# Top-32 attention with two gated feed-forward stages: five places for split output chunks, weight slices one per slot, an early copy on ScalarE, and the experts' first parts between the tail's copies

## Chip, cores and metric

The kernel runs on one core of a Trainium2 chip. The metric is the time of one execution in device microseconds (us), the median of several runs. All data is float32.

## The reference

```python
# attention: q, k, v of [2, 8, 576, 64]
scores = scale * np.matmul(q, k.transpose(0, 1, 3, 2))
kth = np.partition(scores, -32, axis=-1)[..., -32:-31]
scores = np.where(scores >= kth, scores, -1000000000.0)
attn = softmax(scores);  x = attn @ v          # laid out as [1152, 512]
# gated stage: w_a, w_b of [512, 1536], w_out of [1536, 512]
x = ((x @ w_a) * (x @ w_b)) @ w_out
# four experts: w1 of [512, 1024], w2 of [1024, 512] each
p = domain_probs / (domain_probs.sum(-1, keepdims=True) + 1e-09)
out = sum over e of p[:, e:e + 1] * (np.maximum(x @ w1[e], 0.0) @ w2[e])
```

## The kernel before

**Split operands.** The large products run on rounded operands: a tensor is split into an upper part (a ScalarE copy with rounding) and a lower part (whole minus upper, on GpSimd or VectorE), and a product is three matmuls: upper by upper, upper by lower, lower by upper.

**Attention and gated stage, slots 0 to 40.** The 1152 tokens are 9 tiles of 128 (`NT`), the 8 heads 4 pairs (`PR`), which makes 36 pairs of a tile and two heads (`NP`). A loop of slots `n` = 0 to 40 (`LAST`) runs on all engines. In slot n VectorE searches the 32 largest scores of pair n (`top_scores`: per head four MAX8 and three MATCH_REPLACE8, 14 operations, with small work placed between them by `between`). GpSimd makes the limits of pair n-1 (`limits`) and subtracts (`push_down`), ScalarE makes `below_top` and the exponentials, PE transposes (`p_transpose`) and multiplies by v (`weighted_sum`). When the four pairs of a tile are done, VectorE sums and inverts (`sums`), PE turns and spreads the inverses, and VectorE scales the tile (`scale`, operation 10 of the slot, for tile 0 operation 1). The gated stage lags by 5 slots (`LAG_AB`): in slot n PE does the two products `up` of unit n-5, `h_transpose` of unit n-6 behind GpSimd's `product`, and `send` of unit n-7 (nine matmuls of 512 columns with three chunks of w_out). Units 31 to 35 run in the slots 36 to 40 and behind them, without attention beside them: the tail.

**Weights.** w_a and w_b come in eight slices (`SLICES`) by way of three places `w_raw`. Slice i is split by ScalarE (`slice_hi`, L826) in the slot that `HIGH_IN` gives and by GpSimd (L1289 to L1294) in the slot of `LOW_IN`. The twelve chunks of w_out come to `wo_raw` (`RAWS` places), are split in the slots of `CHUNKS_IN` (`chunk_hi`, L831, and L1297 to L1300) into `wo` (`RING` places), written to `wo_d` in DRAM (`keep_chunk`), and read back for each later tile (`reload_chunk`).

**Experts.** 32 steps (`STEPS`): four experts, two groups of tokens, four parts. A step is seven products (`seven`) and `downs`. Step 0 needs the first parts: `w1` parts 0 and 1 split in two instructions each (`w1_high_raws`, `w1_high_sums`, then `w1_low_part` on VectorE), the tokens `x2` in four pieces, and `w2` part 0 (`w2_high`, `w2_low`). PE's order in step 0 is `h_transpose(35)`, `p1 p5 p6 p2 p3 p7`, `send(35)`, `p4`; `p2` waits for ScalarE's eviction of `p1`, `p7` for VectorE's `u2`.

**What sets the order.** Each engine has one instruction stream, written out by hand, and waits on semaphores in that order. SP issues nearly all DMAs, also in order, so a wait of SP holds back all loads behind it.

## Time and profile before

| | |
|---|---|
| median of 3 runs | 818.04 us (817.95 to 818.12) |
| profiled execution, its own time | 818.3 us |
| its span, first to last instruction | 816.5 us |
| PE busy | 775.7 us (95%) |
| VectorE busy | 572.5 us (70%) |
| ScalarE busy | 420.6 us (52%) |
| GpSimd busy | 354.5 us (43%) |
| mean granted TensorE clock | 0.969 |

The page of the profile names the engines PE (TensorE), DVE (VectorE), ACT (ScalarE), POOL (GpSimd) and SP. Busy time is a mean over stretches with different bounds, so the views by stretch and in order of time matter more here. The number in brackets behind a row of a timeline is the idle time of the engine before it, and the arrow names what ended it. The granted clock (PEclk) is the share of full speed: 1.00 is 2.4 GHz, 0.50 is 1.2 GHz.

### The profile page before, as it was taken

How to read it: one execution, taken by the hardware profiler on the slowest of the kernel's cores; microseconds unless marked ns; L12 is line 12 of the kernel's file. 1: busy time of each engine (PE TensorE's matmuls, PEld its weight loads, DVE VectorE, ACT ScalarE, POOL GpSimd, SP SyncE). 2: the span in 40 equal slices, each digit the busy share in tenths (PEclk: the TensorE clock that was granted, in tenths of full speed). 3: DMA queues.
4: the chain of work that ended last, by engine and by line, in shares of the span. 5: the costliest groups of instructions: out<-in, count | busy, mean ns of one | idle time of the engine just before them, and what ended most of it. 6: DMA issues, size and time to landing. Idle time of an engine off the chain costs nothing.

```text
span 816.5 us, 13995 instructions
## 1 busy us (share of the span) xinstructions
PE 775.7 (95%) x5081; PEld 681.4 (83%) x5081; DVE 572.5 (70%) x1145; ACT 420.6 (52%) x818; POOL 354.5 (43%) x322
## 2 busy tenths in 40 slices
PE   4658899999999999999998999999999999999998
PEld 3437778888888888888897898999899999989997
DVE  6989999999999999997627853562455444364423
ACT  3767767777777777776554522342134322343210
POOL 3878775555444444445424302462135521464100
PEclk7569999999999999999999999999999999999999
DMA  7430668444544664544677001300032002210101
GB/s 267 144 118 17 217 230 278 160 166 163 169 169 168 213 226 169 168 156 168 209 247 228 1 26 53 104 27 1 26 104 78 1 1 78 65 65 1 52 1 65
DMA packets 53764, 97.92 MB, mean 120 GB/s; under 512 B 5696, under 2 KB 28992, under 8 KB 53696
## 3 DMA queue, kind: packets, MB, share of 16 engines
q1 hardware_dynamic: 53408, 96.76, 35.3%
q8 instruction: 41, 0.67, 0.3%
q10 hardware_dynamic: 288, 0.26, 0.1%
q14 instruction: 27, 0.22, 0.1%
HBM read 86.00 MB, written 11.01 MB: 119 GB/s over the span
## 4 chain that ended last, share of the span: by engine, by line
PE 83%; DVE 8%; POOL 4%; ACT 3%; issue 2%; ACTq 0%; POOLq 0%; DVEq 0%
PE ps L718 24%; PE ps L650 21%; PE ps L579 15%; PE ps L564 8%; PE ps L528 4%; PE ps L492 4%; PE ps L505 3%; DVE m L1020 2%; PE ps L537 2%; DVE work L1026 2%; POOL wa_lo L1293 1%; POOL p_sb L1250 1%; DVE work L1014 1%; POOL wb_lo L1293 1%; DVE m L1008 1%
## 5 line engine op out<-in xcount | busy, mean ns | idle before, releaser
L1020 DVE MAX8 m<-work 128x8 f32<-128x576 f32 x216 | 152.3, 747 | 0.0
L650 PE MATMUL ps<-x_hi,w_hi 128*128 128x256 f32 (+1 forms) x448 | 133.0, 297 | 3.2 <-DVE u_sb L1128 2.4
L718 PE MATMUL ps<-w_lo,h_hi 128*128 128x512 f32 x288 | 112.8, 392 | 0.0
L718 PE MATMUL ps<-w_hi,h_lo 128*128 128x512 f32 x288 | 112.7, 391 | 0.0
L718 PE MATMUL ps<-w_hi,h_hi 128*128 128x512 f32 x288 | 112.6, 391 | 0.0
L1250 POOL TENSOR_TENSOR p_sb<-s_sb,p_sb 128x576 f32<-128x576 f32 x72 | 101.5, 1428 | 11.7 <-ACT p_sb L770 11.7
L1026 DVE MATCH_REPLACE8 work<-m,work 128x576 f32<-128x576 f32 x144 | 106.0, 743 | 0.0
L1315 POOL TENSOR_TENSOR u_sb<-u_sb,p_sb 128x256 f32<-128x256 f32 (+1 forms) x32 | 31.6, 986 | 161.8 <-DVE u_sb L1141 161.8
L1148 DVE TENSOR_TENSOR c_sb<-ps,p_sb 128x256 f32<-128x256 f32 (+1 forms) x32 | 14.7, 458 | 120.9 <-PE ps L650 120.9
L650 PEld LDWEIGHTS ps<-x_hi,w_hi 128*128 128x128 f32 x448 | 84.6, 189 | 5.4 <-DVE u_sb L1128 2.8
L882 ACT ACTIVATE h_hi<-c_sb 128x256 fp32r<-128x256 f32 (+1 forms) x32 | 14.2, 444 | 120.7 <-DVE c_sb L1148 120.7
L650 PE MATMUL ps<-x_hi,w_raw_lo 128*128 128x256 f32 (+1 forms) x256 | 75.7, 296 | 0.0
L650 PE MATMUL ps<-x_raw_lo,w_hi 128*128 128x256 f32 (+1 forms) x256 | 75.6, 295 | 0.0
L1262 POOL TENSOR_TENSOR hT_lo<-hT_raw,hT_hi 128x384 fp32r<-128x384 f32 x36 | 36.4, 1012 | 86.6 <-ACT hT_raw L813 86.6
L1269 POOL TENSOR_TENSOR h_sb<-a_sb,b_sb 128x384 f32<-128x384 f32 x36 | 37.1, 1031 | 80.3 <-issue 79.8
L564 PE MATMUL ps<-wo,hT_hi 128*128 128x512 f32 x216 | 71.1, 410 | 0.0
L882 ACT ACTIVATE h_hi<-u_sb 128x256 fp32r<-128x256 f32 (+1 forms) x64 | 28.5, 445 | 81.0 <-POOL u_sb L1315 51.0
L1274 POOL TENSOR_TENSOR w_lo<-w_raw,w_hi 128x1024 fp32r<-128x1024 f32 x16 | 39.8, 2488 | 56.1 <-ACT w_hi L863 56.1
L764 ACT ACTIVATE s_sb<-ps 128x576 f32<-128x576 f32 x72 | 46.0, 641 | 34.9 <-POOL p_sb L1250 32.4
L718 PEld LDWEIGHTS ps<-w_hi,h_lo 128*128 128x128 f32 x288 | 54.1, 188 | 11.8
L718 PEld LDWEIGHTS ps<-w_lo,h_hi 128*128 128x128 f32 x288 | 54.1, 188 | 10.7
L718 PEld LDWEIGHTS ps<-w_hi,h_hi 128*128 128x128 f32 x288 | 54.1, 188 | 10.7
(115 smaller groups left out, 2005.8 us busy)
## 6 DMA issues: line engine op xcount, KB each, us to landing
wo<-wo_d SPq DMA_DIRECT2D x96, 512.0 KB, 5.0
w_raw<-moe_w_in SPq DMA_DIRECT2D x32, 256.0 KB, 3.2
w_raw<-moe_w_in SPq DMA_DIRECT2D x16, 512.0 KB, 4.9
wo_d<-wo SPq DMA_DIRECT2D x12, 512.0 KB, 4.5
w_raw<-moe_w_a_in SPq DMA_DIRECT2D x4, 768.0 KB, 5.1
w_raw<-moe_w_b_in SPq DMA_DIRECT2D x4, 768.0 KB, 4.4
wo_raw<-moe_w_out_in SPq DMA_DIRECT2D x12, 256.0 KB, 5.0
x_d<-x_out_sb SPq DMA_DIRECT2D x9, 256.0 KB, 2.4
```

Source lines behind the costliest of these rows:

```text
L564: mm = nc.tensor.matmul(ps_y[:, :], h[:, i, :], wo[g % RING][:, w, :], start=first and j == 0, stop=last and j == 2)
L579: mm = nc.tensor.matmul(bank[:, 0:FS], x[:, t % 2, c, :], w[:, c, cols], start=c == 0 and i == 0, stop=c == DK - 1 and i == 2)
L650: mm = nc.tensor.matmul(ps[:, bank, 0:NH[g]], w, x, start=first and c == n == 0, stop=last and c == HK - 1 and n == 2, skip_group_check=True)
L718: mm = nc.tensor.matmul(ps[:, DOWN_BANKS[j], 0:DM], h[:, f, tok], w[:, f, :], start=m == f == n == 0, stop=m == FM - 1 and f == 1 and n == 2)
L764: copy(s_sb[:, (2 * n + head) % 4, :].rearrange("p (a c) -> p a c", a=2), ps_sc[head], ACT.Copy).then_inc(ac_s, 1)
L882: copy(h_parts[k % 2][0][:, f, j * n:(j + 1) * n], src, ACT.Relu).then_inc(done, 1)
L1020: nc.vector.max(m8[:, par, i, 8 * r:8 * r + 8], work[:, i, :]).then_inc(ve_top, 1)
L1026: nc.vector.match_replace(work[:, i, :], m8[:, par, i, 8 * r:8 * r + 8], work[:, i, :], LOWEST).then_inc(ve_top, 1)
L1250: nc.gpsimd.tensor_tensor(p_sb[:, head, :], s_sb[:, (2 * n + head) % 4, :], p_sb[:, head, :], ALU.subtract).then_inc(po_p, 1)
L1262: nc.gpsimd.tensor_tensor(hT_lo[:], hT_raw[:], hT_hi[:].bitcast(F32), ALU.subtract).then_inc(po_hl, 1)
L1269: nc.gpsimd.tensor_tensor(h_sb[:], a_sb[:], b_sb[:], ALU.mult).then_inc(po_h, 1)
L1274: nc.gpsimd.tensor_tensor(lo[:], whole[:], hi[:].bitcast(F32), ALU.subtract).then_inc(po_w2, 1)
```

## The change

- `RING` 4 to 5 and `RAWS` 5 to 8: five places for split chunks, eight for their sources, four of which lie in the memory of batch 1's v. The wait of chunk 4's load for a slice goes, and v of batch 1 is loaded in slot 10, right behind k, instead of slot 11.
- Slice 0 is copied on ScalarE before the loop; the slots 0 to 3 copy (1, 2), (3, 4), 5, 6, all behind `p_out`; GpSimd's low parts are (0, 1), (2, 3), 4, 5, 6, 7 in the slots 0 to 5.
- The first two of a slot's three chunks are split at the head of the slot on ScalarE, and ahead of `hidden_low` on GpSimd; the third on ScalarE behind `p_out`.
- A tile `zero` is cleared first; PE's eight warming matmuls use it, nine more run ahead of the first `up`, and ScalarE copies it once into `invT` before anything else.
- `sums(1)` moves from operation 1 of slot 9 to operation 12 of slot 8.
- In the tail ScalarE's copies of the experts' first parts are spread: `w1` sums of part 0 behind `b_sb`, `w2_high(0)` in slot 38, pieces of `x2` one at a time, both halves of `w1` part 1 in slot 40 instead of behind the loop. GpSimd makes `w2_low(0)` in two halves in slots 39 and 40, so that `po_w2` counts one more.

```diff
@@ -81,7 +81,6 @@
         p_row = p_sb[:].rearrange("p h s -> p (h s)")
-        top[0] += 4 * H * D
         att_end = top[0]
@@ -95,6 +94,7 @@
         pick = sb("pick", [P, P])
+        zero = sb("zero", [P, P])
@@ -112,15 +112,14 @@
-        RAW, RING, RAWS = 3, 4, 5
+        RAW, RING, RAWS = 3, 5, 8
         ring_at = top[0]
...
         kt1_at = att_at + 4 * PR * S
-        wo_raw = [at(f"wo_raw{i}", [P, DM], F32, (kt1_at if i < 4 else ring_at + 8 * DM * RING - 16 * DM) + 4 * DM * i)
-                  for i in range(RAWS)]
-        assert 16 * DM <= 4 * PR * S
-        top[0] = ring_at + max(4 * DK * FS * RAW, 8 * DM * RING + 4 * DM)
+        wo_raw = [at(f"wo_raw{i}", [P, DM], F32, kt1_at + 4 * DM * i if i < 4 else v1_at + 4 * DM * (i - 4)) for i in range(RAWS)]
+        assert 16 * DM <= 4 * PR * S and 4 * DM * (RAWS - 4) <= 4 * (KC - 1) * H * D
+        top[0] = ring_at + max(4 * DK * FS * RAW, 8 * DM * RING)
@@ -157,8 +156,7 @@
         hi_at += 2 * W2B
-        u2_sb = at("u2_sb", [P, NH[1]], F32, hi_at)
-        assert hi_at + TEMP <= att_end
+        assert hi_at <= att_end
@@ -177,7 +175,9 @@
         late_at += 2 * W2B
+        u2_sb = at("u2_sb", [P, NH[1]], F32, inv_at + TEMP)
         u3_sb = at("u3_sb", [P, NH[1]], F32, inv_at)
+        assert 2 * TEMP <= 4 * DM + 16 * TOP_K
         c21_sb = at("c21_sb", [P, NH[1]], F32, late_at)
@@ -278,7 +278,7 @@
         LAG_AB = 5
-        WARM = 8
+        WARM, FILL = 8, 9
         LAST = NP + LAG_AB - 1
@@ -305,8 +305,8 @@
         SLICES = [(w, c) for c in range(PR) for w in range(2)]
-        HIGH_IN = {0: (0, 1), 1: (2, 3), 2: (4, 5), 3: (6,), 4: (7,)}
-        LOW_IN = {0: (0,), 1: (1, 2), 2: (3, 4), 3: (5,), 4: (6,), 5: (7,)}
+        HIGH_IN = {0: (1, 2), 1: (3, 4), 2: (5,), 3: (6,)}
+        LOW_IN = {0: (0, 1), 1: (2, 3), 2: (4,), 3: (5,), 4: (6,), 5: (7,)}
         CHUNKS_IN = {6: (0, 1, 2), 7: (3, 4, 5), 8: (6, 7, 8), 9: (9, 10, 11)}
@@ -362,9 +362,7 @@
             def load_chunk(g):
-                if g == 4:
-                    sp.wait_ge(po_w, 6)
-                elif g >= RAWS:
+                if g >= RAWS:
                     sp.wait_ge(po_wo, g - RAWS + 1)
@@ -374,7 +372,8 @@
                 sp.wait_ge(pe_w, g - RING + 1)
-                sp.wait_ge(st_wo[g % RING], 16 * (min(g - RING, FO - 1) // RING + 1))
+                for c in {g % FO, min(g - RING, FO - 1)}:
+                    sp.wait_ge(st_wo[c % RING], 16 * (c // RING + 1))
                 sp.dma_start(wo[g % RING][:].rearrange("p a n -> p (a n)").bitcast(F32), wo_d[g % FO]).then_inc(ld_wo[g % RING], 16)
@@ -414,7 +413,6 @@
                     sp.dma_start(kT[:, 1, :, :], k[1].rearrange("r p s -> p r s")).then_inc(ld_k1, 16)
-                if n == 11:
                     load_v(1)
@@ -512,7 +510,7 @@
                     pe.wait_ge(ld_v[0], 48)
-                    pe.wait_ge(ve_z, 3)
+                    pe.wait_ge(ve_z, 4)
                 if n == SPLIT * PR:
@@ -580,10 +578,12 @@
+            def zeros(bank, count):
+                for i in range(count):
+                    nc.tensor.matmul(bank[:, 0:P], zero[:], zero[:], start=True, stop=True)
+
             pe.wait_ge(ve_z, 1)
-            for i in range(WARM):
-                nc.tensor.matmul(ps_b[:, 0:P], x_inv[:].rearrange("p r h -> p (r h)"), x_inv[:].rearrange("p r h -> p (r h)"),
-                                 start=True, stop=True)
+            zeros(ps_b, WARM)
             scores(0)
@@ -619,6 +619,7 @@
                 if m == 0:
+                    zeros(ps_y, FILL)
                     pe.wait_ge(po_xT, 1)
@@ -694,7 +695,7 @@
                 if f == 0 and j == 0 and g == 0:
-                    pe.wait_ge(po_w2, FM * e + m + 1)
+                    pe.wait_ge(po_w2, FM * e + m + 2)
                 if m == 0 and f == 0:
@@ -910,12 +911,17 @@
             load_first_q()
+            act.wait_ge(ve_z, 1)
+            copy(invT[:], zero[:], ACT.Copy)
             scores_out(0, 0)
             scores_out(0, 1)
+            slice_hi(0)
             for n in range(LAST + 1):
...
                     x_hi(0)
+                for g in CHUNKS_IN.get(n, ())[0:2]:
+                    chunk_hi(g)
                 if j is not None:
@@ -934,46 +940,47 @@
                     h_out(u)
+                if m is not None:
+                    act.wait_ge(pe_a, m + 1)
+                    act.wait_ge(po_h, m)
+                    copy(a_sb[:], ps_a[:, 0:FS], ACT.Copy).then_inc(ac_a, 1)
                 if n == NP + 1:
...
                     w1_high_raws(0)
-                    w1_high_sums(0)
                 if n == NP + 2:
-                    x2_high_piece(0, 0)
+                    w2_high(0)
+                if n == NP + 3:
                     x2_high_piece(0, 1)
-                if n == NP + 3:
-                    x2_high_piece(0, 2)
-                    x2_high_piece(0, 3)
-                    w2_high(0)
-                for g in CHUNKS_IN.get(n, ()):
-                    chunk_hi(g)
-                if m is not None:
-                    act.wait_ge(pe_a, m + 1)
-                    act.wait_ge(po_h, m)
-                    copy(a_sb[:], ps_a[:, 0:FS], ACT.Copy).then_inc(ac_a, 1)
-                for i in HIGH_IN.get(n, ())[0:1]:
-                    if n == 1:
-                        slice_hi(i)
+                if n == NP + 4:
+                    w1_high_raws(1)
                 if j is not None:
                     p_out(j)
+                for g in CHUNKS_IN.get(n, ())[2:]:
+                    chunk_hi(g)
                 if scaled_tile(n + 1) is not None:
...
                 for i in HIGH_IN.get(n, ()):
-                    if n < PR and (n, i) != (1, 2):
-                        slice_hi(i)
+                    slice_hi(i)
                 if finished_tile(n) is not None:
...
                     copy(b_sb[:], ps_b[:, 0:FS], ACT.Copy).then_inc(ac_b, 1)
+                if n == NP + 1:
+                    w1_high_sums(0)
+                if n == NP + 2:
+                    x2_high_piece(0, 0)
+                if n == NP + 3:
+                    x2_high_piece(0, 2)
+                    x2_high_piece(0, 3)
+                if n == NP + 4:
+                    w1_high_sums(1)
                 if scaled_tile(n + 1) is not None:
...
             h_out(NP - 1)
-            w1_high_raws(1)
-            w1_high_sums(1)
             p1_out(0)
@@ -1029,13 +1036,14 @@
+            nc.vector.memset(zero[:], 0.0).then_inc(ve_z, 1)
             nc.vector.memset(x_inv[:], 0.0).then_inc(ve_z, 1)
...
                 if t == 0:
-                    dve.wait_ge(ve_z, 1)
+                    dve.wait_ge(ve_z, 2)
                 if t:
@@ -1055,13 +1063,14 @@
             SUMS, SCALE, LOW = 1, 10, 11
-            FIRST_SUMS, FIRST_SCALE = 8, 1
+            FIRST_SUMS, FIRST_SCALE = (8, 12), 1
...
                 t = scaled_tile(n)
-                if n == PR and done == FIRST_SUMS:
-                    sums(0)
-                if t is not None and t > 0 and done == SUMS:
+                for first in range(2):
+                    if n == PR * (first + 1) and done == FIRST_SUMS[first]:
+                        sums(first)
+                if t is not None and t > 1 and done == SUMS:
                     sums(t)
@@ -1268,10 +1277,17 @@
-            def w2_low(q):
+            def chunk_low(g):
+                pool.wait_ge(ac_wo, g + 1)
+                nc.gpsimd.tensor_tensor(wo[g % RING][:, 1, :], wo_raw[g % RAWS][:], wo[g % RING][:, 0, :].bitcast(F32),
+                                        ALU.subtract).then_inc(po_wo, 1)
+
+            def w2_low(q, half=None):
                 pool.wait_ge(ac_w2, q + 1)
                 hi, lo, whole = w2_parts[q % FM]
-                nc.gpsimd.tensor_tensor(lo[:], whole[:], hi[:].bitcast(F32), ALU.subtract).then_inc(po_w2, 1)
+                part = slice(0, 2) if half is None else slice(half, half + 1)
+                nc.gpsimd.tensor_tensor(lo[:, part, :], whole[:, part, :], hi[:, part, :].bitcast(F32),
+                                        ALU.subtract).then_inc(po_w2, 1)
@@ -1292,15 +1308,16 @@
                                             (wa_hi, wb_hi)[w][:, :, cols].bitcast(F32), ALU.subtract).then_inc(po_w, 1)
+                for g in CHUNKS_IN.get(n, ())[0:2]:
+                    chunk_low(g)
                 if u is not None:
                     hidden_low(u)
-                for g in CHUNKS_IN.get(n, ()):
-                    pool.wait_ge(ac_wo, g + 1)
-                    nc.gpsimd.tensor_tensor(wo[g % RING][:, 1, :], wo_raw[g % RAWS][:], wo[g % RING][:, 0, :].bitcast(F32),
-                                            ALU.subtract).then_inc(po_wo, 1)
+                for g in CHUNKS_IN.get(n, ())[2:]:
+                    chunk_low(g)
+                if n - NP - 3 in range(2):
+                    w2_low(0, n - NP - 3)
             product(NP - 1)
             hidden_low(NP - 1)
-            w2_low(0)
```

## Rows read from the trace of the kernel before

**Rows 1.** Windows of the whole span; columns: stretch, length, engines' busy us, PEclk, DMA.

```profile
0.00:63.10 63.10, 35.05 (x198) 24.54 (x198) 52.99 (x113) 38.46 (x58) 40.84 (x40) 0.65 0.50 171
63.10:118.57 55.47, 50.05 (x353) 42.43 (x354) 55.22 (x114) 40.52 (x83) 43.03 (x43) 0.97 0.44 156
118.57:400.00 281.43, 280.94 (x2161) 244.82 (x2162) 259.22 (x539) 202.29 (x408) 138.90 (x160) 1.00 0.54 181
400.00:440.30 40.30, 37.15 (x208) 33.66 (x207) 20.89 (x32) 19.42 (x35) 14.13 (x11) 0.96 0.80 270
440.30:816.50 376.20, 372.52 (x2166) 335.94 (x2164) 184.13 (x350) 119.92 (x236) 117.59 (x70) 1.00 0.14 44
```

**Rows 2.** The chain that ended last, 95 to 130: start us, us, what.

```profile
106.74 0.60 DVE xu L1048
...
112.38 1.56 ACT wo L838 x3
...
115.82 1.38 POOL wo L1299 x2
...
118.57 0.55 PE ps L537 x3
...
121.19 2.11 PE ps L579 x12
```

**Rows 3.** Timelines of ACT and DVE, first 12 us: start, us, instruction [idle before <-releaser].

```profile
7.16 1.28 ACT L764 ACT_TABLE_LOAD   x1 [7.16 <-DVE m L1005]
...
9.21 0.09 DVE L1014 MATCH_VALUE_LOAD work<-m,s_sb 128x8 f32 x1 [1.47 <-ACT s_sb L764]
```

**Rows 4.** Timeline of DVE, 36 to 56 us.

```profile
36.84 1.39 DVE L1008 MAX8 m<-s_sb 128x8 f32<-128x576 f32 x2
...
46.48 1.42 DVE L1008 MAX8 m<-s_sb 128x8 f32<-128x576 f32 x2
...
55.12 0.17 DVE L1035 TENSOR_SCALAR x_den<-x_sum 128x8 f32<-128x8 f32 x1 [3.00 <-ACT p_sb L780]
```

**Rows 5.** Timeline of POOL, 38 to 52 us.

```profile
38.22 3.45 POOL L1293 TENSOR_TENSOR wa_lo<-w_raw,wa_hi 128x1536 fp32r<-128x1536 f32 x1 [1.67 <-ACT wa_hi L829]
41.64 0.20 POOL L1245 TENSOR_SCALAR kbig<-m 128x2 f32<-128x2 f32 x1
...
51.41 2.77 POOL L1250 TENSOR_TENSOR p_sb<-s_sb,p_sb 128x576 f32<-128x576 f32 x2 [1.98 <-ACT p_sb L770]
```

**Rows 6.** Timeline of PE, 1 to 64 us, and the stretch 63.1 to 66.9.

```profile
1.04 3.78 PE L585 MATMUL ps<-x_inv 128*128 128x128 f32 x16 [1.04 <-DVE x_inv L1032]
...
63.10 0.43 PE L579 MATMUL ps<-wa_hi,xT_hi 128*128 128x384 f32 x1 [2.09 <-issue]
...
63.10:66.90 3.80, 3.80 (x13) 3.73 (x14) 3.80 (x8) 2.43 (x6) 3.80 (x3) 0.55 0.00 0
```

**Rows 7.** The tail: timelines of PE and POOL, a stretch, the chain, one line's instructions.

```profile
430.66 0.39 PE L650 MATMUL ps<-x_hi,w_hi 128*128 128x256 f32 x1 [0.77 <-ACT p_sb L870]
...
434.31 0.39 PE L650 MATMUL ps<-x_hi,w_hi 128*128 128x256 f32 x1 [1.95 <-DVE u_sb L1128]
...
435.10:438.70 3.60, 3.60 (x11) 2.79 (x10) 2.74 (x7) 0.13 (x1) 0.85 (x1) 0.54 0.96 323
...
418.74 2.09 PE ps L564 x9
...
419.40 1.02 POOL L1269 TENSOR_TENSOR h_sb<-a_sb,b_sb 128x384 f32<-128x384 f32 x1 [2.81 <-issue]
...
429.71 3.39 POOL L1274 TENSOR_TENSOR w_lo<-w_raw,w_hi 128x1024 fp32r<-128x1024 f32 x1
...
L1111 DVE TENSOR_TENSOR w_sum_lo<-w_sum,w_hi x4: 945/946/3137, 405.1 to 458.9; 128x768 fp32r<-128x768 f32 x4
```

**Rows 8.** The view of DMA issues: KB each, median us from issue to landing.

```profile
wo<-wo_d SPq DMA_DIRECT2D x96, 512.0 KB, 5.0
...
kT<-k_in SPq DMA_DIRECT2D x1, 1152.0 KB, 9.8
```

## Prediction

> **What bounds the kernel now.** I read the stretches first, then the chain of work that ended last, then each engine in order of time around the places where PE stood idle. The stretches [rows 1] say where anything can be won: from 118.57 to 400 PE is busy 280.94 of 281.43 us and DVE only 259.22, so PE is the bound and only less PE work would help; from 440.3 on it is the same until the end. What is left are the first 63.1 us (PE 35.05 busy, at a mean clock of 0.65), the 55.47 us behind them (5.4 us idle) and the tail before the experts, 400 to 440.3 (3.15 us idle). In the second of these DVE is busy 55.22 of 55.47 us: the top-32 search sets the pace there, not PE. The chain [rows 2] hands over in one place: DVE's scaling of tile 1 at 106.74, then a run through ScalarE and GpSimd, and PE from 118.57 on. So whatever moves 118.57 moves the end by as much, since PE works without a gap behind it; and what the tail gains is added to it.
>
> **The early copy on ScalarE.** The first copy of scores meets a table load of 1.28 us at 7.16 [rows 3], in front of everything that DVE does afterwards: DVE's first replacement waits 1.47 us for it and starts at 9.21. With a copy of zeros issued behind the two q loads, the load lies in the first 3 us, where ScalarE has nothing to do. The copy of scores then starts at 7.16 and takes 0.6, DVE goes on at about 7.85 to 7.9: 1.3 us, and it can't be more than the 1.47. The memset of `zero` on DVE is as small as that of `x_inv` beside it and lies long before PE's first scores.
>
> **Slices one per slot.** DVE needs 9.64 us for a pair (36.84 to 46.48, [rows 4]). Its one stall is in pair 4: `sums(0)` waits 3.00 us, until 55.12, for the exponentials of pair 3. These are late because GpSimd was: pair 2 was searched at 36.84, but its limits were made at 41.64 [rows 5], for one low part of a slice is 3.45 us and slot 2 had two (slices 3 and 4), and between the slots GpSimd also waited 1.67 us for the upper half of slice 5. Slots 0 to 3 had 1, 2, 2, 1 low parts and have 2, 2, 1, 1 now. Slot 0 has the room, because slice 0 is now copied before the loop and GpSimd stood idle there until the first upper half. Ahead of the limits of pair 2 one low part goes (3.45) and with it most of the 1.67; the floor is DVE itself, 36.84 - 1.3 = 35.5. I take 36.5 to 38 for the limits of pair 2, some 4 to 5 us earlier; the push of pair 3, at 51.41, and the exponentials behind it come about 3.9 earlier, 55.1 - 3.9 = 51.2. DVE reaches `sums(0)` at 55.12 - 3.00 - 1.3 = 50.8. A stall of 0.4 stays, 2.6 go. DVE from pair 5 on: 1.3 + 2.6 = **3.9 us earlier**. Bounds: 1.3 (the stall stays) and 4.3 (it goes wholly).
>
> **First projection and the nine zero matmuls.** PE's first `up` starts at 63.10 after 2.09 us idle [rows 6]; it hangs on DVE's scaling of tile 0 and moves with DVE, to 59.2. It ran at a granted 0.55, that is nearly all at the lower level of 1.2 GHz, and took 3.8 us for what is 2.11 at the upper one [rows 2, 6]. Eight zero matmuls at the start of the kernel took 3.78 us, 0.47 each; nine are 4.3 at that rate and 2.1 at half of it, the length of the gap. At which level the eight ran their length doesn't tell for sure. If the nine take the shorter time, they end when the operands come, and `up` may keep the clock (1.7 us less on PE); if they take the longer, they put PE back by up to 2.2. PE isn't the bound before 118.57, so I take 0 for both, and keep +2 as the bad end. The Trainium skill (TensorE: Matmul & The Clock Gate, Part 1) holds that the throttled state is the default and that activity lifts it; by that the filling works (the trace agrees so far as the 2.09 us gap is followed by 0.55), and the 1.7 would come to nothing here all the same, as DVE sets the pace.
>
> **Chunks in the slots 6 to 9.** In slot 9 the path from the end of the scaling, 107.34, to PE's start at 118.57 is 11.2 us. It holds three upper copies on ScalarE (1.56) and the rest of three low parts on GpSimd (1.38) [rows 2]. The change puts two of the three at the head of the slot, ahead of `below_top(8,0)`, in time that ScalarE spends waiting for DVE's scaling; so 1.04 of 1.56 leave the path. The third stands behind `p_out` now, and its low part (1.3 us) begins only after it; that leaves the path as long as the 1.38 was, while the waiting for `a_sb`, `p_out` and `b_sb` shrinks by about 0.5. I take **1.5 us**; bounds 0 (the copies move from one wait into another) and 2.9 (both go). In slots 6 to 8 two copies, 1.04 us, are now ahead of `below_top`; what covers them is that GpSimd made its limits late there, being busy with low parts. If that cover were gone, 1.04 in each of four slots, 4.2 us, would stand against this. That `sums(1)` comes three searches earlier (about 2 us) lets PE transpose earlier; the scaling stays at its place in DVE's order, so 0.
>
> **Sync queue and rings.** The wait of chunk 4 for a slice goes, eight sources are loaded at once in slot 3, long before slot 6 reads them: 0. Five places let a reload go one chunk earlier; PE never waits for one now (its idle time from 118.57 to 400 is 0.5 us): 0. V of batch 1 is loaded in slot 10, so the reloads of slot 11 stand behind it; see the last rival.
>
> **The tail.** PE idles 0.77 and 1.95 us [rows 7]: ScalarE makes the experts' second upper part before it evicts `p1`, and DVE then makes two low parts, the second of 3.14 us, before `u2`, on which `p7` waits. Behind the gap `send(35)` ran at a granted 0.54, 3.60 us for what is 2.09 at the upper level. With the upper part in slot 40, and its low parts on DVE right behind, where DVE had nothing to do, all this goes: 0.77 + 1.95 + 1.51 = **4.2 us**. Next late is the eviction of `p1`, which ScalarE can start right behind `h_out(35)`, while PE works on its first three products until 430.66 - 0.77 = 429.9. `w2_low(0)` goes in halves between `hidden_low` and the next `product`, where GpSimd idled 2.8 us; a half is at most 1.7 (half of 3.39), so 0. Bounds of the tail: 1.5 and 4.7.
>
> **A rule against it.** The 3.14 us of that low part, the longest of four whose median is 0.95, fell together with GpSimd's 3.39 us instruction at 429.71 [rows 7]. The Trainium skill (SBUF — State Buffer, on the shared port pair) says that GpSimd and a DVE instruction with two SBUF inputs exclude each other for a whole instruction; the trace agrees with it by these two rows. The change takes this clash off the path and puts two smaller ones into slots 39 and 40.
>
> **Sum.** 3.9 + 1.5 + 4.2 = 9.6 us. The profiled execution took 818.3 (span 816.5), 0.3 above the median of 818.04. From 818.3 this gives 808.7, from the median 808.4, which I predict; the span should be about 806.9.
>
> **Rivals.**
> 1. The stall at `sums(0)` stays: slice 0 lands too late for its early place, or ScalarE's two upper copies in slots 0 and 1 hold up `below_top`. For it: ScalarE is in order. Against it: DVE is one pair ahead in those slots. Only 1.3 of 3.9 come: 818.04 - 1.3 - 1.5 - 4.2 = 811.0.
> 2. The tail gives less: halves of `w2_low(0)` meet DVE's low parts, so that `product` in slot 40 and behind the loop is late by up to 1.2 each, and PE waits: 4.2 - 2.4 = 1.8; 818.04 - 5.4 - 1.8 = 810.8. Against it: 2.8 us of room.
> 3. Chunk copies ahead of `below_top` cost their 4.2: 818.04 - 9.6 + 4.2 = 812.6; with rival 1 on top 815.2.
> 4. It doesn't do what it says: the table load comes again at the first use, the stall only moves, and PE's tail waits for other low parts: 818.
> 5. Slower. K and V of batch 1 are issued together in slot 10, 9.8 us for K [rows 8] and, by its size, at most as much for V. The three reloads of slot 11 stand behind both, 5.0 each: 19.6 + 15 = 34.6 us if all lands one after another, against two slots, 20.8, until `send` needs them. PE would wait 13.8: 818.04 - 9.6 + 13.8 = 822.2. It decides from the point at which the transfers take more than two slots; it is slower than before if they take over 30.4. Against it: the medians are of overlapped transfers, and the DMA share from 118.57 to 400 is 0.54 [rows 1].
>
> **How the numbers follow.** Forecast 0.60 (808.4, from 806 to 810.5), rival 1 0.15, rival 2 0.11, rival 3 0.06, rival 4 0.03, rival 5 0.05. The range must reach to rivals 1 and 2: 805.8 to 812.4. A difference of 0.2% (1.6 us) is about what a measurement of this kernel can tell from none. Faster by more: the first four cases, 0.92 less a little for a sum of two rivals, 0.91; same 0.04; slower 0.05.
>
> **What would show it.** Right: the table load before 3 us; DVE's first replacement at 7.9; the wait before `x_den` under 1 us and `x_den` at 51.2; the first `up` at about 59.2; `h_transpose` of slot 10 at 113.1, with PE busy to over 99.5% behind it; no gap before `p2` and `p7`, and `send(35)` in 2.1 us at full clock. Wrong: a wait of ScalarE for a slice's load before 12 us; `x_den` at 53.8 or later (rival 1); GpSimd's `product` late in the tail with PE's `h_transpose` behind it (2); PE waiting in `send` for a reload near 130 (5).

## The result and the profile after

| | before | after |
|---|---|---|
| median | 818.08 us (817.95 to 819.17, 4 runs) | **808.45 us** (807.91 to 809.39, 4 runs) |
| ratio to before, 95% interval | | 0.9881 [0.9863, 0.9898] |
| profiled execution, its own time | 818.3 us | 809.39 us |
| its span | 816.5 us | 807.6 us |
| mean granted TensorE clock | 0.969 | 0.977 |

The median fell by 9.6 us, to within 0.1 us of the forecast. The span of the profiled execution, the longest of the four, fell by 8.9. I read the same places in the same order as for before. First the stretches, cut at the same events as in [rows 1], and then two short ones in slot 4 (stretch, length, engines' busy us, PEclk, DMA):

```profile
0.00:59.00 59.00, 35.19 (x198) 24.86 (x199) 51.64 (x109) 36.97 (x57) 39.51 (x38) 0.68 0.55 196
59.00:112.90 53.90, 48.99 (x353) 41.48 (x355) 53.67 (x113) 41.45 (x85) 42.76 (x40) 1.00 0.42 152
112.90:391.00 278.10, 277.62 (x2138) 241.81 (x2135) 260.63 (x541) 201.64 (x407) 139.70 (x163) 1.00 0.54 183
391.00:431.40 40.40, 40.40 (x255) 37.03 (x254) 20.52 (x36) 21.59 (x39) 13.73 (x13) 1.00 0.75 245
431.40:807.60 376.20, 372.29 (x2164) 335.72 (x2162) 184.35 (x350) 119.84 (x236) 117.57 (x70) 1.00 0.15 46
50.30:53.30 3.00, 2.63 (x10) 1.86 (x10) 2.97 (x9) 2.02 (x6) 1.55 (x1) 0.50 0.00 0
53.80:57.00 3.20, 3.14 (x28) 2.52 (x28) 2.58 (x4) 0.17 (x1) 1.78 (x3) 0.50 0.00 0
```

The fourth row is the tail: PE busy 40.40 of 40.40 us at full clock, where it idled 3.15 before. The last two rows lie in slot 4, and there the clock was at its lower level. In before's profile it was at its upper one: v's product took 1.31 us, against 2.40 below.

```profile
57.30 1.31 PE L528 MATMUL ps<-pT,v_sb 128*64 128x128 f32 x20 [0.69 <-ACT pT L788]
```

ScalarE in the first 12 us (start, us, instruction [idle before <-releaser]). The table load lies at 1.64 now and the first copy of scores takes its time alone:

```profile
1.64 1.28 ACT L915 ACT_TABLE_LOAD   x1 [1.64 <-PEq L1357]
2.94 0.31 ACT L915 ACTIVATE invT<-zero 128x128 f32<-128x128 f32 x1
7.46 1.31 ACT L765 ACTIVATE s_sb<-ps 128x576 f32<-128x576 f32 x2 [4.22 <-DVE m L1012]
```

VectorE: its first maxima, the first replacement, `x_den` and `xu` of tile 0, `xu` of tile 1. There is no wait ahead of `x_den`, and one of 1.38 us ahead of the first `xu`, which before's profile didn't have:

```profile
6.60 1.43 DVE L1012 MAX8 m<-ps 128x8 f32<-128x576 f32 x2 [4.71 <-PE ps L490]
8.22 0.09 DVE L1021 MATCH_VALUE_LOAD work<-m,s_sb 128x8 f32 x1 [0.19 <-ACT s_sb L765]
...
51.11 0.17 DVE L1043 TENSOR_SCALAR x_den<-x_sum 128x8 f32<-128x8 f32 x1
...
57.76 0.69 DVE L1056 TENSOR_TENSOR xu<-ps,inv_b 128x512 f32<-128x512 f32 x1 [1.38 <-ACT inv_b L799]
...
104.21 0.67 DVE L1056 TENSOR_TENSOR xu<-ps,inv_b 128x512 f32<-128x512 f32 x1
```

PE from slot 4 on: a gap of 2.54 us, then transposes and v's product at the lower level, the nine zero matmuls, the first `up`, the `up` that needs tile 1, and `h_transpose` of slot 10:

```profile
50.37 1.12 PE L503 MATMUL ps<-ident,p_sb 128*128 128x128 f32 x4 [2.54 <-ACT p_sb L781]
...
53.85 2.40 PE L526 MATMUL ps<-pT,v_sb 128*64 128x128 f32 x20 [0.58 <-ACT pT L789]
...
58.88 2.27 PE L583 MATMUL ps<-zero 128*128 128x128 f32 x18
60.97 0.44 PE L577 MATMUL ps<-wa_hi,xT_hi 128*128 128x384 f32 x1
...
106.33 0.45 PE L577 MATMUL ps<-wa_hi,xT_hi 128*128 128x384 f32 x1 [1.66 <-DVE xT_lo L1062]
...
114.75 0.55 PE L535 MATMUL ps<-ident,h_sb 128*128 128x128 f32 x3
```

GpSimd in the tail: the two halves of `w2_low(0)`, and the products `h_sb` behind each, 1.6 us after the half has ended. From slot 38 on each product takes 1.02 us here:

```profile
412.13 1.28 POOL L1289 TENSOR_TENSOR w_lo<-w_raw,w_hi 128x512 fp32r<-128x512 f32 x1
415.03 1.02 POOL L1278 TENSOR_TENSOR h_sb<-a_sb,b_sb 128x384 f32<-128x384 f32 x1 [1.61 <-issue]
...
418.74 1.28 POOL L1289 TENSOR_TENSOR w_lo<-w_raw,w_hi 128x512 fp32r<-128x512 f32 x1
421.63 1.02 POOL L1278 TENSOR_TENSOR h_sb<-a_sb,b_sb 128x384 f32<-128x384 f32 x1 [1.61 <-issue]
```

In before the product of slot 38 took 1.80 us, beside a low part on VectorE, and PE waited 0.43 us for it:

```profile
405.10 1.80 POOL L1269 TENSOR_TENSOR h_sb<-a_sb,b_sb 128x384 f32<-128x384 f32 x1 [2.82 <-issue]
```

```profile
406.96 0.55 PE L537 MATMUL ps<-ident,h_sb 128*128 128x128 f32 x3 [0.43 <-POOL h_sb L1269]
```

And the low parts of `w_sum` on VectorE (min, median, max ns), the longest of which was 3137 in [rows 7]:

```profile
L1120 DVE TENSOR_TENSOR w_sum_lo<-w_sum,w_hi x4: 945/1074/1203, 402.0 to 450.0; 128x768 fp32r<-128x768 f32 x4
```

`send(35)` runs from 427.54 to 429.6, behind `p7` with no gap.

### The profile page after: what moved, and what is told of

It reads as the page before. It is cut to its first block, busy times and chain, and to the rows that moved or that the text cites. A ratio compares the mean times of both kernels' runs of the same rounds, so it can differ in the third digit from the quotient of the medians.

```text
span 807.6 us, 14033 instructions
## 1 busy us (share of the span) xinstructions
PE 774.5 (96%) x5099; PEld 680.9 (84%) x5099; DVE 570.8 (71%) x1146; ACT 421.5 (52%) x819; POOL 353.3 (44%) x323
## 4 chain that ended last, share of the span: by engine, by line
PE 85%; DVE 6%; ACT 3%; POOL 3%; issue 3%; ACTq 0%; POOLq 0%; DVEq 0%
PE ps L719 24%; PE ps L651 21%; PE ps L577 17%; PE ps L562 8%; PE ps L526 4%; PE ps L490 4%; PE ps L503 4%; PE ps L535 2%; DVE m L1027 2%; DVE work L1033 1%; POOL p_sb L1259 1%; POOL wb_lo L1309 1%; DVE work L1021 1%; DVE m L1015 1%; PE ps L546 1%
## 5 line engine op out<-in xcount | busy, mean ns | idle before, releaser
L883 ACT ACTIVATE h_hi<-u_sb 128x256 fp32r<-128x256 f32 (+1 forms) x64 | 28.5, 445 | 79.1 <-POOL u_sb L1332 51.2
L1289 POOL TENSOR_TENSOR w_lo<-w_raw,w_hi 128x1024 fp32r<-128x1024 f32 (+1 forms) x17 | 39.0, 2294 | 54.8 <-ACT w_hi L864 54.8
```

The lines of the kernel that those rows point to most:

```text
L883: copy(h_parts[k % 2][0][:, f, j * n:(j + 1) * n], src, ACT.Relu).then_inc(done, 1)
L1289: nc.gpsimd.tensor_tensor(lo[:, part, :], whole[:, part, :], hi[:, part, :].bitcast(F32), ALU.subtract).then_inc(po_w2, 1)
```

## The experiments

In the ratios to the kernel before, each of which has before's own runs on the same chip, the differences from the changed kernel can be read: a step of 0.0012 is 1 us. The changed kernel stands at 0.98825, the mean of its two measurements.

| kernel | median us | ratio [95%] | against the changed kernel |
|---|---|---|---|
| `again`, the changed kernel | 808.90 | 0.9884 [0.9871, 0.9898] | |
| `no_early_copy` | 809.99 | 0.9899 [0.9885, 0.9912] | +1.4 |
| `old_slices` | 810.83 | 0.9906 [0.9891, 0.9922] | +1.9 |
| `chunks_behind` | 810.75 | 0.9908 [0.9894, 0.9921] | +2.1 |
| `old_tail` | 813.19 | 0.9932 [0.9918, 0.9945] | +4.1 |
| `no_fill` | 808.87 | 0.9881 [0.9866, 0.9896] | -0.1 |
| `five_sources_v_later` | 808.70 | 0.9886 [0.9873, 0.9900] | +0.3 |
| `ring_of_four` | 816.44 | 0.9975 [0.9965, 0.9986] | +7.6 |
| `ring_four_chunks_behind` | 811.62 | 0.9917 [0.9904, 0.9931] | +2.8 |
| `tail_alone` (before and the new tail) | 814.57 | 0.9939 [0.9926, 0.9953] | -5.0 from before |
| `hold_slot4` | 808.06 | 0.9867 [0.9854, 0.9880] | -1.3 |
| `hold_slots1to4` | 807.62 | 0.9860 [0.9847, 0.9874] | -1.8 |

Each interval is about 1.1 us to either side, and a difference of two kernels has the error of both, so 0.3 is nothing, 1.4 is not clear of noise by the ratios alone, and 1.9 and 2.1 are barely so; where the rows show the same step, they carry the reading. Taken back alone, early copy, slices, order of the chunks and tail cost 1.4 + 1.9 + 2.1 + 4.1 = 9.5 us, against the change's 9.6. With an error of over 1 us in each term, that the sum comes so near is chance; what it shows is that these four make up most of the change. No run takes back the earlier `sums(1)` alone, for which the prediction had 0.

**The changed kernel again.**

> The changed kernel once more, beside the others, as their common anchor. Expected: 9.6 us below the kernel before (808.5), wait of DVE before x_den 0, wait of DVE for inv_b about 1.4, PE's h_transpose of slot 10 at about 114.8. If the position of the clock's fall ahead of slot 4 differs from one execution to the next, single executions should lie at two or three levels within 807.9 to 809.4.

808.90 us, but the rows were not those expected: `h_transpose` of slot 10 came at 113.75, 1.0 earlier than in the first profile, and the profiled span was 806.6. VectorE waited 0.52 us ahead of `x_den` (at 52.06) and not at all ahead of `xu`, for slot 4 ran at the upper level:

```profile
54.24 1.31 PE L526 MATMUL ps<-pT,v_sb 128*64 128x128 f32 x20 [0.68 <-ACT pT L789]
```

So the wait ahead of `xu` comes in some executions of one and the same kernel. The single executions lay between 808.15 and 809.56.

**Without the early copy.**

```diff
-            act.wait_ge(ve_z, 1)
-            copy(invT[:], zero[:], ACT.Copy)
```

> The changed kernel without the copy of zeros on ScalarE. Theory (steps of the prediction): the table load stands in front of the first copy of scores again, DVE starts 1.3 late and stays so, x_den at 52.4, and the end is 1.3 us later, 809.8. Rival (the load is hidden by then): DVE waits 1.38 us for inv_b in slot 5 of the changed kernel, so a DVE that is 1.3 late only uses this up, and the end moves by 0.3 or less, 808.5 to 808.8.

+1.4 us, as the theory had it. VectorE's first rows show the term itself. From its start to the replacement are 2.90 us, 1.62 in the changed kernel; the difference is 1.28, the table load:

```profile
5.96 1.43 DVE L1010 MAX8 m<-ps 128x8 f32<-128x576 f32 x2 [4.07 <-PE ps L490]
8.86 0.09 DVE L1019 MATCH_VALUE_LOAD work<-m,s_sb 128x8 f32 x1 [1.47 <-ACT s_sb L765]
```

**The slices as before.** The core of the edit; the copy of slice 0 goes back into the loop as well:

```diff
-        HIGH_IN = {0: (1, 2), 1: (3, 4), 2: (5,), 3: (6,)}
-        LOW_IN = {0: (0, 1), 1: (2, 3), 2: (4,), 3: (5,), 4: (6,), 5: (7,)}
+        HIGH_IN = {0: (0, 1), 1: (2, 3), 2: (4, 5), 3: (6,), 4: (7,)}
+        LOW_IN = {0: (0,), 1: (1, 2), 2: (3, 4), 3: (5,), 4: (6,), 5: (7,)}
```

> The changed kernel with the slices where they were (slots 0 to 4 upper, 0 to 5 lower, none before the loop). Both theories expect the stall before x_den back, 2.6 to 3.0 us. Theory A (the stall's worth goes through whole): 2.6 us slower, 811.1. Theory B (about half of the gain was lost to the lower clock of PE between x_inv and inv_b, and comes back when the clock is up in slot 4 as it was before): scaling of tile 0 at about 59.0 against 57.8, 1.2 us slower, 809.7.

+1.9 us, between the two theories. The stall is back in full. From the first maxima (6.18 here) `xu` came 2.4 us later than in the changed kernel's first profile, for its wait for `inv_b` was 0.63 here instead of 1.38, and 3.4 later than in `again`, which had no such wait. So how much of the stall reaches `xu` depends on the execution:

```profile
53.85 0.17 DVE L1046 TENSOR_SCALAR x_den<-x_sum 128x8 f32<-128x8 f32 x1 [3.00 <-ACT p_sb L781]
...
59.75 0.69 DVE L1059 TENSOR_TENSOR xu<-ps,inv_b 128x512 f32<-128x512 f32 x1 [0.63 <-ACT inv_b L799]
```

**The tail as before.** The core of the edit:

```diff
                 if n == NP + 1:
                     w1_high_raws(0)
+                    w1_high_sums(0)
...
             h_out(NP - 1)
+            w1_high_raws(1)
+            w1_high_sums(1)
             p1_out(0)
```

> The changed kernel with the tail's copies and the low part of w2 as before. Theory: the gaps of 0.8 and 1.9 us, send(35) at the lower clock (1.5) and the 0.4 to 0.6 before h_transpose of slot 38 are back: 4.2 to 5.1 slower, 812.7 to 813.6. Rival (part of it is given back in steps 1 and 2, where DVE is late anyway): 3 us or less, 811.5.

+4.1 us, just under the theory's 4.2 to 5.1, and PE's three waits of before are back at their places:

```profile
401.76 0.55 PE L535 MATMUL ps<-ident,h_sb 128*128 128x128 f32 x3 [0.42 <-POOL h_sb L1273]
...
425.51 0.39 PE L651 MATMUL ps<-x_hi,w_hi 128*128 128x256 f32 x1 [0.77 <-ACT p_sb L871]
...
429.15 0.39 PE L651 MATMUL ps<-x_hi,w_hi 128*128 128x256 f32 x1 [1.95 <-DVE u_sb L1132]
429.96 0.63 PE L562 MATMUL ps<-wo,hT_hi 128*128 128x512 f32 x2
```

The last row is `send(35)`. In this execution its first pair took 0.63 and the whole ran at the upper level, though the gap of 1.95 stood ahead of it as in before, where the clock then fell [rows 7]. From `h_transpose` of slot 10 to the end of the span were 810.0 - 113.35 = 696.7 us here, 697.9 in before and 692.9 in the changed kernel. So the gaps and what stands by them cost 3.8 in this profile, and before's, in which the clock fell, is 1.3 longer. What lies behind the last `h_transpose` (427.26 in before, 422.10 here, 422.90 in the changed kernel) took 389.2, 387.9 and 384.7 us: the two gaps cost 3.2, more than their idle 2.72, and the remaining 0.5 to 0.6 was lost ahead of it, at the wait for `h_sb`.

**The new tail alone, in the kernel before.**

> The kernel before with the tail's new order alone (ScalarE's copies spread, w2's low part in two halves), with four places for chunks. Theory A (the parts add up): 4.3 us faster than the kernel before, as putting the old tail back cost 4.3. Theory B (the fifth place belongs to the tail as well: in the run with four places send(35) waited 0.74 and 0.35 us for reloads once PE reached it earlier): only 3 to 3.5 us faster, with waits of PE on a reload ahead of or within send(35).

-5.0 us from before (814.57 to 819.06, 4.5 by the medians), against 4.1 when it is taken out of the changed kernel: within the error of some 1.5 us the parts add up. From `h_transpose` of slot 10 to the end the profile has 693.1 us, 4.9 less than before's. With four places and no gap ahead of `send(35)`, PE waited there 0.17 us for a reload.

**Without the nine zero matmuls.**

```diff
-        WARM, FILL = 8, 9
+        WARM, FILL = 8, 0
```

> The changed kernel without the nine zero matmuls ahead of the first up. Theory: up of unit 0 runs at the lower clock and ends 1.7 us later on PE, but VectorE sets the pace until slot 9, so the end moves by 0.3 us or less (against 808.5 to 808.9 of the changed kernel), and PE's gaps in slots 5 to 7 shrink by what up takes longer. Rival: PE is the bound from slot 5 on, and the end is 1.7 us later.

No difference, as the theory had it. The first `up` met the lower level behind a gap of 2.05 us and took 0.52 us for an instruction that takes 0.33 in the changed kernel:

```profile
61.20 0.66 PE L577 MATMUL ps<-wa_hi,xT_hi 128*128 128x384 f32 x1 [2.05 <-issue]
61.66 0.52 PE L577 MATMUL ps<-wa_lo,xT_hi 128*128 128x384 f32 x1
```

The filling does what it says, and it buys nothing, for VectorE sets the pace there: from `xu` of tile 0 to `h_transpose` of slot 10 it is 57.0 us in this profile and in the changed kernel's. Nor do the nine matmuls hurt when they run long: in the profile of `old_tail` they took 3.96 us, and the same stretch was 56.7.

**The chunks behind, as before.** The core of the edit; GpSimd's low parts of the chunks go behind `hidden_low` in the same way:

```diff
-                for g in CHUNKS_IN.get(n, ())[0:2]:
-                    chunk_hi(g)
...
                 if u is not None:
                     h_out(u)
+                for g in CHUNKS_IN.get(n, ()):
+                    chunk_hi(g)
```

> The changed kernel with all three copies of chunks behind h_out on ScalarE and behind hidden_low on GpSimd, as before. Theory: from the end of the scaling of tile 1 to h_transpose of slot 10 it takes 11.2 us again instead of 9.9, the end is 1.3 to 1.5 later, 810.0. Rival: the copies only move from one wait into another, 0, and h_transpose comes as early as in the changed kernel.

+2.1 us, where the theory had 1.3 to 1.5. `xu` of tile 1 starts at 103.19, 1.0 earlier than in the changed kernel's first profile (and where `again` has it, 103.21), and yet `h_transpose` of slot 10 comes 0.3 later (1.3 later than in `again`), behind a wait that had gone. From the end of the scaling to it are 115.09 - 103.87 = 11.2 us, as in before; in the changed kernel 114.75 - 104.88 = 9.9:

```profile
115.09 0.55 PE L535 MATMUL ps<-ident,h_sb 128*128 128x128 f32 x3 [0.53 <-POOL h_sb L1276]
```

**Four places.**

```diff
-        RAW, RING, RAWS = 3, 5, 8
+        RAW, RING, RAWS = 3, 4, 8
```

> The changed kernel with four places for split chunks, all else as changed. The prediction put the fifth place at 0, from PE never waiting for a reload. Theory A (that holds): 0. Theory B (the fifth place is what lets the copies go to the head of the slot: with four, the copy of chunk 4 at the head of slot 7 waits for PE's first chunk of send in the same slot, likewise in slots 8 and 9, and below_top, the push and the exponentials stand behind it): 1.5 to 4 us slower, with ScalarE idle 1 to 3 us before its copies of chunks in slots 7 to 9, released by PE's send.

+7.6 us, the largest cost of any part, which I had put at 0 in the prediction. It is theory B's mechanism, at nearly twice its upper bound of 4. ScalarE at the head of the slots 7, 8 and 9 (the second and third arrows are given as issue; that they are the same wait is read from the length and from PE, whose `send` begins at 93.67 and 108.27):

```profile
80.75 0.63 ACT L839 ACTIVATE wo<-wo_raw 128x512 fp32r<-128x512 f32 x1 [2.63 <-PE ps L562]
...
94.69 0.63 ACT L839 ACTIVATE wo<-wo_raw 128x512 fp32r<-128x512 f32 x1 [2.63 <-issue]
...
109.29 0.63 ACT L839 ACTIVATE wo<-wo_raw 128x512 fp32r<-128x512 f32 x1 [2.49 <-issue]
```

The copy of chunk 4 needs the place of chunk 0, which `send(0)` of the same slot reads; on PE that `send` stands late in the slot (its first pair at 79.72). ScalarE is in order, so the exponentials are held up behind the copy, and VectorE behind them:

```profile
99.81 0.32 DVE L1043 TENSOR_SCALAR x_den<-x_sum 128x8 f32<-128x8 f32 x1 [5.58 <-ACT p_sb L781]
```

`h_transpose` of slot 10 comes at 120.95, 6.2 later than in the changed kernel. The rest is in the tail, where PE waits for reloads inside `send(35)`, 0.74 us and then 0.35:

```profile
435.32 0.73 PE L562 MATMUL ps<-wo,hT_hi 128*128 128x512 f32 x2 [0.74 <-DMA wo<-wo_d]
```

With five places the two copies at the head need no `send` of their own slot: 3 and 4 go to places not used yet, and 6 and 7, 9 and 10 to places whose chunks were sent in the slot before.

**Four places and the chunks behind.** The edits of the last two together.

> Of the changed kernel this takes back two parts together: four places instead of five, and all three chunk copies of a slot stand on ScalarE where they stood before (behind h_out, ahead of a_sb), low parts on GpSimd behind hidden_low. Taking back the order alone gave +1.9 us, taking back the fifth place alone +7.6. The chunk g needs the place of chunk g-4; the first two chunks of a slot at the head of the slot then wait for a send that PE makes late in the same slot; behind h_out it is near that send anyway. Theory A, the fifth place is only what the early copies need: with the copies behind, four places cost nothing in the slots 6 to 9, DVE's x_den of tile 1 has no wait of over 1 us, and at most 0.2 to 1.1 us come from reloads in the tail, where send(35) now starts earlier: 1.9 to 3.0 above the changed kernel, ratio to the kernel before about 0.991 to 0.993. Theory B, the fifth place is worth its own time in any order: ScalarE's waits of 2.6 us for a send stay, and the costs add up to 7.6 + 1.9 = 9.5 us, ratio 1.000.

+2.8 us, 0.7 over the order alone: theory A. ScalarE's three copies follow one another without a wait (first row), `h_transpose` of slot 10 is where `chunks_behind` had it, and only the tail's wait for reloads is left:

```profile
95.86 1.68 ACT L839 ACTIVATE wo<-wo_raw 128x512 fp32r<-128x512 f32 x3
```

```profile
115.23 0.55 PE L535 MATMUL ps<-ident,h_sb 128*128 128x128 f32 x3 [0.54 <-POOL h_sb L1276]
...
429.81 0.74 PE L562 MATMUL ps<-wo,hT_hi 128*128 128x512 f32 x2 [0.95 <-DMA wo<-wo_d]
431.12 0.74 PE L562 MATMUL ps<-wo,hT_hi 128*128 128x512 f32 x2 [0.34 <-DMA wo<-wo_d]
```

So the fifth place and the early copies are one step. Together they are worth 2.8 us; the early copies without the place lose 4.8 (7.6 - 2.8). With the copies behind, what the place itself is worth lies in the tail alone: 0.7 by the ratios, 1.7 by the profiles of this run and `chunks_behind` from slot 10 to the end (694.5 and 692.8), which the noise doesn't tell apart.

**Five sources, v one slot later.**

```diff
-        RAW, RING, RAWS = 3, 5, 8
+        RAW, RING, RAWS = 3, 5, 5
...
+                if n == 11:
                     load_v(1)
```

> The changed kernel with five places for chunk sources instead of eight, and v of batch 1 loaded in slot 11 again. Theory: 0, within 0.3 us. Rival 5 of the prediction (the reloads of slot 11 behind k and v of batch 1): faster than the changed kernel, and PE's send of slot 12 would show a wait in the changed one, which it doesn't.

No difference (+0.3), as the theory had it.

**Holding the clock in slot 4, and in the slots 1 to 4.** More zero matmuls on PE ahead of the transposes; the second kernel has {1: 20, 2: 16, 3: 2, 4: 9} for {4: 9}:

```diff
+        HOLD = {4: 9}
...
+                    zeros(ps_y, HOLD.get(n, 0))
                     p_transpose(n - 1, None)
```

> The changed kernel with nine more zero matmuls ahead of p_transpose in slot 4, where PE idles 2.5 us and the granted clock falls in some executions. Theory A (the lower clock between x_inv and inv_b costs DVE its wait of up to 1.4 us): v's product in slot 4 takes 1.31 instead of 2.40, DVE's wait for inv_b goes, tile 0 is scaled about 1.4 us earlier in the executions that had the fall, and the median goes down by 0.5 to 1.4 us. Theory B (the wait is due to the order of ScalarE's work, not the clock): no change.

> The changed kernel with zero matmuls ahead of p_transpose in slots 1 to 4 (20, 16, 2 and 9). Theory A: PE is at the upper clock for most of the first 60 us, the spread between executions shrinks, x_den is not stalled in any, and the median is 1 to 2 us below the changed kernel's. Theory B: VectorE sets the pace and the fills last twice as long at the lower clock, so they hold PE back: 0, or up to 1 us slower.

With slot 4 alone, -1.3 us by the ratios, but only 0.4 to 0.8 by the medians (808.06 against 808.45 and 808.90): not clear of noise. Nor does the profile show the reason as I had it. The transposes ran at the upper level (0.66), which they also did, behind the gap of 2.54 us, in three profiles without the added matmuls, and v's product was at the lower one all the same, behind two gaps of 0.7. The wait ahead of `xu` was 0.67:

```profile
50.23 0.66 PE L504 MATMUL ps<-ident,p_sb 128*128 128x128 f32 x4 [0.35 <-ACT p_sb L783]
51.63 0.63 PE L504 MATMUL ps<-ident,p_sb 128*128 128x128 f32 x4 [0.74 <-ACT s_sb L767]
53.16 2.25 PE L527 MATMUL ps<-pT,v_sb 128*64 128x128 f32 x20 [0.68 <-ACT pT L791]
```

With the slots 1 to 4 filled, -1.8 us by the ratios, 0.8 to 1.3 by the medians: the lowest median here, and hardly clear of noise. The mean granted clock was 0.987 to 0.989 in all four executions, against 0.972 to 0.977 in the eight of the changed kernel, so the filling raised it every time. From 50 to 60 us the clock was 1.00, against 0.66 in the changed kernel's profile, and neither `x_den` nor `xu` waits:

```profile
50.00:60.00 10.00, 7.85 (x71) 6.75 (x72) 9.97 (x22) 6.37 (x11) 7.13 (x6) 1.00 0.00 0
```

```profile
5.70 1.43 DVE L1014 MAX8 m<-ps 128x8 f32<-128x576 f32 x2 [3.81 <-PE ps L491]
...
50.11 0.17 DVE L1045 TENSOR_SCALAR x_den<-x_sum 128x8 f32<-128x8 f32 x1
...
55.29 0.68 DVE L1058 TENSOR_TENSOR xu<-ps,inv_b 128x512 f32<-128x512 f32 x1
```

That its first maxima came at 5.70 is not the edit's doing, for it lies ahead of all added matmuls.

## Why the prediction held, step by step

**Two misses of size cancelled.** The head came to 3.8 us instead of 5.4 in the profiled execution, the tail to 5.1 instead of 4.2. The table splits the span in four, by VectorE's rows and `h_transpose` of slot 10 (before had its first maxima at 6.31 and its first `xu` at 60.30):

| profile | start of the first maxima | from there to `xu` of tile 0 | from there to slot 10 | from there to the end |
|---|---|---|---|---|
| before | 6.31 | 53.99 | 58.27 | 697.9 |
| forecast | same | -3.9 | -1.5 | -4.2 |
| after | +0.29 | -2.83 | -1.28 | -5.1 |
| `again` | +0.73 | -3.79 | -1.76 | -5.1 |
| `hold_slots1to4` | -0.61 | -4.40 | -1.72 | -5.2 |

*Early copy, 1.3.* Right: 1.28 by the rows, 1.4 by the run without it.

*Slices, 2.6, and "DVE from pair 5 on: 3.9 us earlier".* The stall shrank from 3.00 to nothing in the first profile and to 0.52 in `again`, where a rest of 0.4 was forecast, so the argument by GpSimd's two low parts held. (`x_den` at 51.11 where 51.2 was forecast is in part chance: the stall went wholly, and the start was 0.29 later.) What the sum left out is the next link. `xu` needs the inverses that PE turns and spreads behind v's product, and how long that takes goes with the clock of slot 4, in all fourteen profiles:

| PE in slot 4 | profiles | `x_den` to `xu` | wait ahead of `xu` |
|---|---|---|---|
| v's product 1.31 us | before, `again`, `chunks_behind`, `ring_four_chunks_behind`, `hold_slots1to4` | 5.18 us | none |
| v's product 2.21 to 2.40, transposes 0.66 | seven others, `tail_alone` among them | 5.90 to 6.09 | 0.63 to 0.82 |
| v's product 2.40, transposes 1.1 | after, `no_early_copy` | 6.65 | 1.38 to 1.39 |

At the upper level the two terms together were 3.8 us, as forecast; in the first profile they were 2.8. It isn't the change that brings the wait: `tail_alone`, which has before's head, shows it too, and its own stall of 2.99:

```profile
55.51 0.17 DVE L1040 TENSOR_SCALAR x_den<-x_sum 128x8 f32<-128x8 f32 x1 [2.99 <-ACT p_sb L780]
...
61.59 0.69 DVE L1053 TENSOR_TENSOR xu<-ps,inv_b 128x512 f32<-128x512 f32 x1 [0.82 <-ACT inv_b L798]
```

So part of the miss of 1.6 at the head compares an execution of before at the upper level with one of the changed kernel at the lower. The prediction asked at which level the zero matmuls and `up` would run, and didn't ask it of slot 4. Together with the later start it is also most of the reason why the first `up`, forecast at 59.2, came at 60.97.

*Chunks, 1.5.* Right in size (1.4 from the end of the scaling to `h_transpose`, 1.3 and 1.8 by the table, 2.1 by the run), and in place: the 11.2 us of before became 9.9, and 11.2 again with the copies behind. That two copies ahead of `below_top` cost nothing (rival 3 falls) held only because of the fifth place. **The step that failed in its reasoning is "Five places let a reload go one chunk earlier ... 0".** I looked at who waits for a reload, and the place's first user isn't a reload but ScalarE's own copy, which waits for the `send` that frees it. It didn't hurt the number, since the change has both halves, but a reader who left out the ring "worth 0" would have lost 7.6 of 9.6 us. The range would not have held that kernel, whose runs lay between 813.9 and 817.2.

*Nine zero matmuls, 0.* Right. They took 2.27 us in this profile, the short one of the two lengths, and `up` kept its clock, with no gain.

*Queue, rival 5, 0.05.* Fell: no wait for a reload near 130 us, and v one slot later changes nothing.

*Tail, 4.2.* The mechanism was right and the size 0.9 too small; the parts are read from before's profile, the changed kernel's and that of `old_tail`. The two gaps, put at their idle time of 2.72, cost 3.2 from start to start. The wait for `h_sb` in slot 38, 0.43 us in before, is a third one, which I hadn't priced, though it is in the 3.15 us of idle time that [rows 1] gives for the tail; about 0.5 went there. A low part on VectorE lay beside GpSimd's product and stretched it to 1.80 (1.02 now). This is the exclusion of the Trainium skill (SBUF — State Buffer, on the shared port pair) once more; the trace agrees by this pair and by the 3.14 us low part that is 1.20 at most now. The two smaller clashes that the prediction put into the slots 39 and 40 don't show: the halves of `w2_low(0)` end at 413.41 and 420.02, before VectorE's next low parts start at 413.79 and 420.40. The clock behind the gap, put at 1.51, was 1.3, and it is not a sure term: `old_tail` had the gap and kept the clock in its profiled execution. Rivals 1, 2 and 4 fell with the rows above.

**By chance or not.** That the forecast came within 0.1 us is luck: an error of 1.6 one way and 0.9 the other left 0.7, and the rest lies in where the executions fall. The median of after is 0.9 below its profiled execution, as the median of before is 0.2 below its own. The range (805.8 to 812.4) holds all four runs.

**What stays open.** Why the clock fell in slot 4 in some executions and not in others is not settled. That v's product ran at the upper level with the slots 1 to 4 filled is seen in one profile, and four profiles without the filling have it too; whether its 1.8 us come from there or in part from where the start fell, these runs don't tell.

## What to carry to other kernels

Before a place in a ring is priced at nothing, ask for each copy into it which read frees the place, and in which slot that read stands: work that is moved ahead of such a read on an in-order engine needs enough places that none of them waits for the read. Here two copies ahead of `send` needed five where four had done. Where a stall is taken out, follow the chain to the next operand that the same engine needs, and ask at which clock the engine that makes it runs. And make a part's price by taking it back alone from the finished kernel: here four parts made up the change within the noise, and one that seemed free was the condition of another. Two profiles of one kernel can differ by 1 us in one place, so look at a second one before a miss of that size is put down to the change.

## What the hardware showed unexpectedly

**Single executions differ by more than most parts of this change.** The medians of before lay between 818.1 and 819.1 in five sets of runs, its single runs between 817.2 and 819.7. Part of it stands in the rows. VectorE's first maxima wait for PE's first scores, and these started at the same time, 4.75 us, in most profiles but took from 1.24 to 2.29 us, the lengths that they have at the upper and the lower level; so the first maxima started between 5.70 and 7.09 us in the fourteen profiles, and what VectorE does next is shifted by as much. Two more places ran at 1.2 GHz in some executions and at 2.4 GHz in others: slot 4 of the head, which was worth up to 1.5 us ahead of `xu`, and `send(35)` behind before's gap of 1.95 us, worth 1.3. Behind one and the same gap of 2.54 us in slot 4 the transposes took 1.12 us in one profile and 0.66 in three (`old_tail`, `five_sources_v_later`, `ring_of_four`). So a gap of about 2 us on PE was followed by the lower level sometimes, and not always; a forecast should take its cost as a bound and not as a term. The Trainium skill (TensorE: Matmul & The Clock Gate, Part 1) says that the slow matmuls at a kernel's start vary in number and length between runs of one kernel; the trace agrees by the eight score matmuls, 1.80 us in the first profile of the changed kernel and 2.23 in `again`.
